# Bias part of a fused attention and MoE kernel: the fourth group of features of nine sets is made by GpSimd instead of VectorE

## The chip, the cores and the metric

The program runs on one core of one Trainium2 chip. The time is the device time of one execution in microseconds (us). The kernel is written engine by engine: each engine has its own instruction stream, and semaphores order them.

The names in the profile are PE for TensorE (PEld for its weight loads), DVE for VectorE, ACT for ScalarE, POOL for GpSimd and SP for the engine that only issues DMAs here.

## The reference

Three stages follow each other: attention with a learned bias by position, a dense layer pair, and a mixture of eight experts with one expert chosen per token. Only the first stage is touched:

```python
B, H, S, D = q.shape                       # 4, 8, 576, 64; hidden = 32
scores = scale * np.matmul(q, k.transpose(0, 1, 3, 2))
rel = (pos[:, None] - pos[None, :]).astype(np.float32)
psi_rel = np.log1p(np.abs(rel))
psi_i = np.log1p(np.maximum(pos[:, None].astype(np.float32), 1.0))
x = (psi_rel / psi_i)[..., None]
h = np.maximum(x @ w1 + b1, 0.0)           # 576 x 576 x 32
bias = h @ w2                              # 576 x 576 x 8
scores = scores + bias.transpose(2, 0, 1)[None, :, :, :]
```

The hidden layer h has 32 features for each pair of a query and a key, and is the same for all four batches. The softmax, the product with v, the dense stage and the experts follow.

## The kernel before

**What the bias part computes.** The 576 queries are cut in 36 sets of 16. A set has four groups of four queries. For one group, the 128 partitions hold 4 queries times 32 features, and the 576 columns are the keys. Since 1/psi_i is positive, it is taken out of the ReLU: a feature is max(w1 * psi_rel, -b1 * psi_i) plus a part that does not depend on the key, or relu(w1 * psi_rel + b1 * psi_i). The first form is one DVE tensor_scalar (a max against one number per partition, L630), the second one ACT activation (L543). Both read a window of 576 columns of the tile dist_sb (128x1148, f32) and write one of the four slots of a feature buffer feat, which has three buffers (NF = 3), 128x4x576 f32 each.

**Who makes which group.** DVE makes groups 0, 1 and 2 of each set (ACT_GROUP = 3). Group 3 is made by ACT in the sets where by_scalar(s) holds, s % 4 != 3, which are 27 sets, and by DVE in the other nine (s = 3, 7, ..., 35). So DVE makes 27*3 + 9*4 = 117 features.

**What follows a set.** TensorE multiplies the four slots by the 128x32 matrix w2_blk, 8 products of 288 columns (L401; the profile has each as two records, so a set is 16). It waits for feat_v (DVE's groups), for feat_a where ACT made one, and for acc_read, since the results alternate between two pairs of PSUM banks. ACT then scales the result into a row buffer (bias_rows, L553, for the last two sets L556), and SP stores it to DRAM (L332). The bias comes back from DRAM in tiles (L339) when the first scores of the attention need it.

**What sets the order.** Everything around the change is written out by hand, one loop over s per engine. DVE makes the features of set s after acc_ready says that TensorE has used the buffer of set s-3. ACT makes its group of set s+2 and then the rows of set s. Between sets, ACT and DVE also split the first k and q into high and low parts (L564; L639 and L642, five places). TensorE computes the first scores, scores(0, 0) at L420, between the last two sets. DVE then adds the bias to them (L657). GpSimd has no work in this part: its first own instruction is an indirect DMA of the routing, at 514.65 us of the span.

Of the kernel before, what the change touches and what calls it, by code (L numbers as in the profile page):

```python
# [23 lines left out]
ALU = mybir.AluOpType  # L24
# [16 lines left out]
SETS = S // SET  # L41
# [30 lines left out]
class Attention:  # L72
# [2 lines left out]
    tensor: object  # L75
    scalar: object
    vector: object
    over: object
    banks_read: object
    turned: object  # L80
# [73 lines left out]
def bias_and_attention(nc, stay, mem, w1, b1, w2, dist, psi, rpsi_rows, bias_dram, q, k, v, ident, x_dram):  # L154
# [7 lines left out]

    with ExitStack() as ctx:
        def sem(name):
            return stay.enter_context(nc.semaphore("at_" + name))

        def buf(name, shape, dt=F32):
            return ctx.enter_context(nc.sbuf_tensor("at_" + name, shape, dt))  # L170
# [6 lines left out]
        NF, NR = 3, 7  # L177
        ACT_GROUP = 3
        TILE_SETS = P // SET

        feat = [buf(f"feat{i}", [P, 4, S]) for i in range(NF)]
# [18 lines left out]
        lower, upper = buf("lower", [P, S // GQ]), buf("upper", [P, S // GQ])  # L200
# [14 lines left out]
        dist_scaled, b1_negated, bounds_set = sem("dist_scaled"), sem("b1_negated"), sem("bounds_set")  # L215
        shift_done, shift_zeroed, shift_read = sem("shift_done"), sem("shift_zeroed"), sem("shift_read")
        table_in = sem("table_in")
        feat_v, feat_a = sem("feat_v"), sem("feat_a")
        acc_ready, acc_read = sem("acc_ready"), sem("acc_read")
        rows_out = [sem(f"rows_out{i}") for i in range(NR)]  # L220

# [23 lines left out]
        def by_scalar(s):  # L245

            return s % 4 != 3

        def by_scalar_upto(s):

            return s + 1 - (s + 1) // 4

        def acc(s):

            if s < SETS - 2:
                return [score[s % 2][:, half, 0:HALF] for half in range(2)]
            return [bank[:, 0:HALF] for bank in ((pt_a, pt_b) if s == SETS - 2 else (o_acc, misc))]

        def window(s, c):
            return dist_sb[:, DIST0 - (4 * s + c) * GQ:DIST0 - (4 * s + c) * GQ + S]  # L260

        def column(t, s, c):
            return t[:, 4 * s + c:4 * s + c + 1]
# [125 lines left out]
        def tensor(pe, dense):  # L389
            def bias_set(s):  # L390
                pe.wait_ge(feat_v, s + 1)
                if by_scalar(s):
                    pe.wait_ge(feat_a, by_scalar_upto(s))
                if 2 <= s < SETS - 2:
                    pe.wait_ge(acc_read, s - 1)
                if s == SETS - 1:
                    pe.wait_ge(shift_read, 2)
                    pe.wait_ge(lo_done, NP)
                for half in range(2):
                    for c in range(4):  # L400
                        last = nc.tensor.matmul(acc(s)[half][c * 32:(c + 1) * 32, :], w2_blk[:, :],  # L401
                                                feat[s % NF][:, c, half * HALF:(half + 1) * HALF], start=True, stop=True)
                last.then_inc(acc_ready, 1)
# [78 lines left out]
            for s in range(SETS):  # L482
                bias_set(s)
                if s == SETS - 2:
                    scores(0, 0)
# [139 lines left out]
        def vector(dve, dense):  # L625
            def features(s):
                if s >= NF:
                    dve.wait_ge(acc_ready, s - NF + 1)
                for c in range(ACT_GROUP if by_scalar(s) else 4):
                    last = nc.vector.tensor_scalar(feat[s % NF][:, c, :], window(s, c), column(lower, s, c), None, ALU.max)  # L630
                last.then_inc(feat_v, 1)

# [85 lines left out]
            for s in range(SETS):  # L718
                features(s)
                if s - 4 in EARLY:  # L720
                    low(0, EARLY[s - 4])
# [39 lines left out]
            scaled(LASTP, 0, QT - 1, misc, 0)  # L761
            scaled(LASTP, QT - 1, 1, pt_a, 0)

        return Attention(sync, tensor, scalar, vector, over, banks_read, turned)

# [1269 lines left out]
def build(nc, io):  # L2037

    def scratch(name, shape, dt=F32):
        return nc.dram_tensor(name, shape, dt, kind="Internal").ap()  # L2040

    bias_dram = scratch("bias_dram", (S * NH, S))
    x_dram = scratch("x_dram", (DM, TOK))
    x2_dram = scratch("x2_dram", (TOK + 1, DM))
    slot_dram = scratch("slot_dram", (P * SLOT_COLS, 2), I32)
    with (nc.sbuf_tensor("ctl", [1, CTL], I32) as ctl, nc.sbuf_tensor("first_ctl", [1, 3 + NTT], I32) as first_ctl,
          nc.sbuf_tensor("slot_i", [P, NTT], I32) as slot_i, nc.sbuf_tensor("slot_rows", [P, NTT, 2], I32) as rows_sb):
        with ExitStack() as stay:
            def bank(name, shape):
                return stay.enter_context(nc.psum_tensor(name, shape, F32))  # L2050

            def buf(name, shape):
                return stay.enter_context(nc.sbuf_tensor(name, shape, F32))

            mem = Shared(buf("id_sb", [P, P]), stay.enter_context(nc.semaphore("id_in")),
                         [bank(f"score{c}", [P, 2, BANK]) for c in range(2)], bank("pt_a", [P, BANK]), bank("pt_b", [P, BANK]),
                         bank("misc", [P, BANK]), bank("o_acc", [P, BANK]), buf("minus_b", [P, 1]), buf("minus_small", [P, 1]),
                         buf("ones", [P, P]), buf("seen", [P, 2 * CH, NE]))
            first = bias_and_attention(nc, stay, mem, io["w1"], io["b1"], io["w2"], io["dist"], io["psi"], io["rpsi_rows"],
                                       bias_dram, io["q"], io["k"], io["v"], io["ident"], x_dram)  # L2060
            then = dense_and_routing(nc, stay, mem, first, ctl, first_ctl, slot_i, rows_sb, io["moe_w_in"], io["moe_w_out"],
                                     io["moe2_w_gate"], io["before"], io["token_ids"], io["down"], io["upto"],
                                     io["bases"], io["count"], io["empty"], io["zeros"], x_dram, x2_dram,
                                     slot_dram)
            last = experts(nc, stay, mem, then, ctl, first_ctl, io["moe2_w1"], io["moe2_w2"], x2_dram, slot_dram, io["out"])
            with nc.Block() as block:
                @block.sync
                def _(sp):
                    first.sync(sp, then)
                    then.sync(sp, last)  # L2070

                @block.tensor
                def _(pe):
                    first.tensor(pe, then)
                    then.tensor(pe, last)

                @block.scalar
                def _(act):
                    first.scalar(act, then)
                    then.scalar(act, last)  # L2080

                @block.vector
                def _(dve):
                    first.vector(dve, then)
                    then.vector(dve, last)

                @block.gpsimd
                def _(pool):
                    then.gpsimd(pool, last)


# [16 lines left out]
```

## Time and profile before

| | |
|---|---|
| median of 3 executions | 1054.19 us (1054.02 to 1054.94) |
| the profiled execution | 1053.72 us, of which the span of the profile is 1051.8 us |
| PE busy | 1012.9 us (96%) |
| DVE busy | 689.2 us (66%) |
| ACT busy | 631.2 us (60%) |
| POOL busy | 87.3 us (8%) |
| bias part | from the start to about 59.4 us of the span |

The span runs from the first to the last instruction of the profile; about 1.9 us of the execution lie outside it. The shares are means over stages that are limited by different engines. What the change is worth has to be read from the first 60 us, where TensorE is less busy than later and DVE more. Consecutive instructions of one engine overlap at their ends in the records (the next starts before the last one's results have landed), so the distance from start to start is shorter than the duration of one.

### The profile page before, as it was taken

How to read it: one execution, taken by the hardware profiler on the slowest of the kernel's cores; microseconds unless marked ns; L12 is line 12 of the kernel's file. 1: busy time of each engine (PE TensorE's matmuls, PEld its weight loads, DVE VectorE, ACT ScalarE, POOL GpSimd, SP SyncE). 2: the span in 40 equal slices, each digit the busy share in tenths (PEclk: the TensorE clock that was granted, in tenths of full speed). 3: DMA queues.
4: the chain of work that ended last, by engine and by line, in shares of the span. 5: the costliest groups of instructions: out<-in, count | busy, mean ns of one | idle time of the engine just before them, and what ended most of it. 6: DMA issues, size and time to landing. Idle time of an engine off the chain costs nothing. (4 is left out here: it accounts for less than half of the span.)

```text
span 1051.8 us, 19004 instructions
## 1 busy us (share of the span) xinstructions
PE 1012.9 (96%) x6540; PEld 787.9 (75%) x6540; DVE 689.2 (66%) x1570; ACT 631.2 (60%) x1340; POOL 87.3 (8%) x134
## 2 busy tenths in 40 slices
PE   6889999999999999999999999999998999999995
PEld 2256666666665789988988989888877888888884
DVE  7987878787888896766757657668754442632321
ACT  6987777777777685666566556567732432732421
POOL 0000000000000000000100100001023231331221
PEclk9999999999999999999999999999999999999998
DMA  7771252422512530010100100201115351631111
GB/s 227 265 250 56 71 168 71 160 81 65 148 46 94 183 111 1 31 31 31 31 1 31 31 1 31 81 31 58 40 51 205 122 195 40 215 102 40 36 40 36
DMA packets 62094, 92.15 MB, mean 88 GB/s; under 512 B 24486, under 2 KB 29990, under 8 KB 61990
## 3 DMA queue, kind: packets, MB, share of 16 engines
q1 hardware_dynamic: 56806, 79.32, 22.9%
q0 software_dynamic: 4192, 11.07, 3.3%
q8 instruction: 52, 0.85, 0.3%
q10 hardware_dynamic: 1008, 0.61, 0.2%
q14 instruction: 36, 0.29, 0.1%
HBM read 66.19 MB, written 25.73 MB: 87 GB/s over the span
## 5 line engine op out<-in xcount | busy, mean ns | idle before, releaser
L1009 PE MATMUL score<-dl_xt,dl_weights 128*128 128x384 f32 x1152 | 219.8, 339 | 0.0
L1009 PEld LDWEIGHTS score<-dl_xt,dl_weights 128*128 128x128 f32 x1152 | 202.1, 188 | 8.5 <-issue 3.0
L574 ACT ACTIVATE at_prob<-at_neg,at_negmax 128x576 f32<-128x576 f32 (+1 forms) x160 | 123.6, 773 | 54.2 <-DVE at_negmax L657 40.2
L1169 ACT ACTIVATE dl_val<-score 128x384 f32<-128x384 f32 x96 | 47.1, 490 | 131.3 <-PE score L1009 125.9
L1261 DVE SCALAR_TENSOR_TENSOR dl_sq<-dl_sq,dl_val 128x384 f32<-128x384 f32 x96 | 53.5, 557 | 99.3 <-ACT dl_sq L1171 97.7
L657 DVE CUSTOM_DVE_ANT_0 at_neg<-score,at_bias 128x576 f32<-128x576 f32 (+1 forms) x160 | 114.2, 750 | 2.2 <-PE score L420 1.7
L1814 PE MATMUL o_acc<-dl_weights,ex_ht_hi 128*128 128x512 f32 x336 | 109.1, 405 | 0.9 <-ACT ex_y_sb L1899 0.9
L1784 PE MATMUL score<-dl_weights,ex_xt_hi 128*128 128x512 f32 x336 | 105.6, 395 | 0.0
L435 PE MATMUL o_acc<-at_prob_t,at_v_nat 128*64 128x512 f32 (+1 forms) x320 | 85.7, 616 | 1.2 <-DVE at_o_sb L693 1.2
L428 PEld LDWEIGHTS pt_b<-id_sb,at_prob 128*128 128x128 f32 (+1 forms) x320 | 32.0, 140 | 63.5 <-ACT at_prob L574 48.1
L1479 POOL DMA_INDIRECT slot_dram<-slot_rows,slot_i x18 | 17.8, 987 | 727.5 <-DVE slot_i L1342 723.9
L1784 PEld LDWEIGHTS score<-dl_weights,ex_xt_hi 128*128 128x128 f32 x336 | 61.5, 188 | 12.2 <-issue 0.2
L1814 PEld LDWEIGHTS o_acc<-dl_weights,ex_ht_hi 128*128 128x128 f32 x336 | 60.0, 188 | 12.5 <-ACT ex_y_sb L1899 1.1
L1814 PE MATMUL o_acc<-dl_weights,ex_ht_lo 128*128 128x512 f32 x168 | 66.2, 394 | 0.0
L1784 PE MATMUL score<-dl_weights,ex_xt_lo 128*128 128x512 f32 x168 | 65.7, 391 | 0.0
L1054 PE MATMUL o_acc<-dl_weights,dl_g_hi 128*128 128x512 f32 x192 | 60.6, 396 | 1.9 <-DVE dl_g_lo L1257 1.6
L1171 ACT ACTIVATE dl_sq<-dl_val,minus_b 128x384 f32<-128x384 f32 x96 | 59.3, 618 | 3.1
L420 PE MATMUL score<-at_k_hi,at_q_hi 64*128 64x288 f32 x320 | 58.0, 340 | 2.6 <-DVE at_negmax L657 2.0
L1272 DVE COPY_PREDICATED dl_sq<-dl_over,dl_big 128x384 f32<-128x384 uint32 x96 | 57.8, 602 | 3.5 <-DVE dl_sq L1268 0.2
L1054 PE MATMUL score<-dl_weights,dl_g_hi 128*128 128x512 f32 x192 | 59.8, 392 | 0.0
L1054 PE MATMUL pt_b<-dl_weights,dl_g_hi 128*128 128x512 f32 x192 | 59.3, 390 | 0.0
L1179 ACT ACTIVATE dl_over<-dl_val,minus_small 128x384 f32<-128x384 f32 x96 | 58.2, 606 | 0.0
(222 smaller groups left out, 1985.8 us busy)
## 6 DMA issues: line engine op xcount, KB each, us to landing
dl_raw<-in_moe_w SPq DMA_DIRECT2D x12, 1024.0 KB, 7.6
ex_raw_b<-in_moe_w SPq DMA_DIRECT2D x8, 1024.0 KB
at_bias<-bias_dram SPq DMA_DIRECT2D x3, 2304.0 KB, 10.2
bias_dram<-at_prob SPq DMA_DIRECT2D x20, 288.0 KB, 2.1
at_k_all<-in_k SPq DMA_DIRECT2D x16, 288.0 KB, 3.5
at_q_all<-in_q SPq DMA_DIRECT2D x16, 288.0 KB, 4.2
at_v_nat<-in_v SPq DMA_DIRECT2D x16, 288.0 KB, 3.1
bias_dram<-at_rows_sb SPq DMA_DIRECT2D x16, 288.0 KB, 3.6
```

The lines of the kernel that those rows point to most:

```text
L420: last = nc.tensor.matmul(score[c][:, half, 0:HALF], a[g % 2][part, cols], b[g % 2][part, keys], start=i == 0, stop=i == 2)
L435: last = nc.tensor.matmul(o[c * D:(c + 1) * D, at:at + queries.stop - queries.start], v_nat[g % NV][keys, j, :], prob_t[g % 2][keys, j, qu ...
L574: nc.scalar.activation(prob[n % 2][0:m, c, :], neg[c][n % 2][0:m, :], ACT.Exp, bias=negmax[c][n % 2][0:m, 0:1], scale=-1.0, accum_out=tota ...
L657: nc.vector.tensor_tensor_reduce(out=neg[c][n % 2][0:m, :].rearrange("p (a c) -> p a c", a=2), in0=score[c][0:m, :, 0:HALF], in1=bias[hp % ...
L1009: last = nc.tensor.matmul(h_ps[m % NHB][:, 0:CN], w[f // KT][:, k, fc], x[c % 2][:, k, :], start=k == 0 and n == 0, stop=k == KT - 1 and n ...
L1054: last = nc.tensor.matmul(x2_ps[j][:, :], g[m % 2][:, tok], w[f // KT][:, f % KT, :], start=f == 0 and n == 0, stop=f == FT - 1 and n == 2)
L1171: nc.scalar.activation(sq[m % 2][:, :], val[m % 2][:, :], ACT.Square, bias=minus_b[:, 0:1], scale=SQ_A).then_inc(sq_done, 1)
L1179: nc.scalar.activation(over[m % 2][:, :], val[m % 2][:, :], ACT.Relu, bias=minus_small[:, 0:1]).then_inc(over_done, 1)
L1261: nc.vector.scalar_tensor_tensor(out=sq[m % 2][:, :], in0=sq[m % 2][:, :], scalar=SQ_C, in1=val[m % 2][:, :], op0=ALU.add, op1=ALU.mult).t ...
L1272: nc.vector.copy_predicated(s[:, :], over[m % 2][:, :].bitcast(mybir.dt.uint32), big[m % 2][:, :]).then_inc(dve_step, 1)
L1784: last = nc.tensor.matmul(h_ps[half][:, :], x[:, k, :], w1_of(r, half, w)[:, k, :], start=k == 0 and n == 0, stop=k == KT - 1 and n == 2)
L1814: last = nc.tensor.matmul(y_ps[:, :], x[:, half * KT + k, :], weights[:, r % 2, half, w, k, :], start=half == 0 and k == 0 and n == 0, sto ...
```

## The change

GpSimd gets an instruction stream for the bias part. In the nine sets of which ACT makes no group, it makes group 3, by the same tensor_scalar with the same operands that DVE had. DVE makes three groups of every set. TensorE waits for a new semaphore, feat_g, in these nine sets. GpSimd waits for the same two semaphores at the start as DVE, and for acc_ready before it writes to a buffer that was used before, which all nine were.

```diff
-        feat_v, feat_a = sem("feat_v"), sem("feat_a")
+        feat_v, feat_a, feat_g = sem("feat_v"), sem("feat_a"), sem("feat_g")
...
                 pe.wait_ge(feat_v, s + 1)
                 if by_scalar(s):
                     pe.wait_ge(feat_a, by_scalar_upto(s))
+                else:
+                    pe.wait_ge(feat_g, s + 1 - by_scalar_upto(s))
...
-                for c in range(ACT_GROUP if by_scalar(s) else 4):
+                for c in range(ACT_GROUP):
                     last = nc.vector.tensor_scalar(feat[s % NF][:, c, :], window(s, c), column(lower, s, c), None, ALU.max)
                 last.then_inc(feat_v, 1)
...
+        def gpsimd(pool):
+
+            pool.wait_ge(dist_scaled, 1)
+            pool.wait_ge(bounds_set, 2)
+            for s in range(SETS):
+                if not by_scalar(s):
+                    if s >= NF:
+                        pool.wait_ge(acc_ready, s - NF + 1)
+                    nc.gpsimd.tensor_scalar(feat[s % NF][:, ACT_GROUP, :], window(s, ACT_GROUP), column(lower, s, ACT_GROUP), None,
+                                            ALU.max).then_inc(feat_g, 1)
...
                 def _(pool):
+                    first.gpsimd(pool)
                     then.gpsimd(pool, last)
```

On DVE, in sets 0 to 5 of the bias part, the program before has these rows (at_feat0 to at_feat2 are the three feature buffers; x2 stands for two in a row):

```order
L630 TENSOR_SCALAR at_feat0<-at_dist_sb,at_lower 128x576 [waits at_bounds_set,at_dist_scaled]
L630 TENSOR_SCALAR at_feat0<-at_dist_sb,at_lower 128x576 x2
L630 TENSOR_SCALAR at_feat1<-at_dist_sb,at_lower 128x576 x3
L630 TENSOR_SCALAR at_feat2<-at_dist_sb,at_lower 128x576 x3
L630 TENSOR_SCALAR at_feat0<-at_dist_sb,at_lower 128x576 [waits at_acc_ready]
L630 TENSOR_SCALAR at_feat0<-at_dist_sb,at_lower 128x576 x3
L630 TENSOR_SCALAR at_feat1<-at_dist_sb,at_lower 128x576 [waits at_acc_ready]
L630 TENSOR_SCALAR at_feat1<-at_dist_sb,at_lower 128x576 x2
```

The same place on DVE in the changed program:

```order
L634 TENSOR_SCALAR at_feat0<-at_dist_sb,at_lower 128x576 [waits at_bounds_set,at_dist_scaled]
L634 TENSOR_SCALAR at_feat0<-at_dist_sb,at_lower 128x576 x2
L634 TENSOR_SCALAR at_feat1<-at_dist_sb,at_lower 128x576 x3
L634 TENSOR_SCALAR at_feat2<-at_dist_sb,at_lower 128x576 x3
L634 TENSOR_SCALAR at_feat0<-at_dist_sb,at_lower 128x576 [waits at_acc_ready]
L634 TENSOR_SCALAR at_feat0<-at_dist_sb,at_lower 128x576 x2
L634 TENSOR_SCALAR at_feat1<-at_dist_sb,at_lower 128x576 [waits at_acc_ready]
L634 TENSOR_SCALAR at_feat1<-at_dist_sb,at_lower 128x576 x2
```

Set 3, the second use of at_feat0, has three instructions now where it had four, and the same holds for each fourth set after it. On GpSimd the changed program has, between the constants at its start and the first DMA of the routing, which stood next to each other before:

```order
L2113 MEMSET const-uint8-127 128x1
L2102 UNCONDITIONAL_BRANCH [waits barrier_Pool_Activation_PE_DVE_SP_gather]
L776 ISA
L776 TENSOR_SCALAR at_feat0<-at_dist_sb,at_lower 128x576 [waits at_acc_ready,at_bounds_set,at_dist_scaled]
L776 TENSOR_SCALAR at_feat1<-at_dist_sb,at_lower 128x576 [waits at_acc_ready]
L776 TENSOR_SCALAR at_feat2<-at_dist_sb,at_lower 128x576 [waits at_acc_ready]
```

Nine instructions moved there, for sets 3, 7, 11 and so on, with nothing else between them. On TensorE only the wait of set 3 and its like changes; before, sets 3 and 4 begin with

```order
L401 MATMUL score1<-at_feat0,at_w2_blk 32x288 [waits at_acc_read,at_feat_v]
L401 MATMUL score1<-at_feat0,at_w2_blk 32x288 x7
L401 MATMUL score0<-at_feat1,at_w2_blk 32x288 [waits at_acc_read,at_feat_a,at_feat_v]
L401 MATMUL score0<-at_feat1,at_w2_blk 32x288 x7
L401 MATMUL score1<-at_feat2,at_w2_blk 32x288 [waits at_acc_read,at_feat_a,at_feat_v]
```

and in the changed program with

```order
L405 MATMUL score1<-at_feat0,at_w2_blk 32x288 [waits at_acc_read,at_feat_g,at_feat_v]
L405 MATMUL score1<-at_feat0,at_w2_blk 32x288 x7
L405 MATMUL score0<-at_feat1,at_w2_blk 32x288 [waits at_acc_read,at_feat_a,at_feat_v]
L405 MATMUL score0<-at_feat1,at_w2_blk 32x288 x7
L405 MATMUL score1<-at_feat2,at_w2_blk 32x288 [waits at_acc_read,at_feat_a,at_feat_v]
```

The products of set 3 wait for GpSimd too; no instruction of TensorE moves.

## Rows read from the trace of the kernel before

**Rows 1.** Stretches of the span: busy us (instructions) by engine, clock, DMA

```profile
14.00:24.00 10.00, 8.90 (x128) 3.81 (x120) 10.00 (x24) 10.00 (x15) 0.00 (x0) 1.00 0.60 227
24.00:57.00 33.00, 26.44 (x365) 9.56 (x366) 33.00 (x81) 30.50 (x48) 0.00 (x0) 1.00 0.76 258
```

**Rows 2.** Waits, 24 to 57 us: total, times, longest us

```profile
PEld score L401 <- DVE at_feat L630: 18.8, 23, 1.4
PE score L401 <- DVE at_feat L630: 5.1, 10, 0.8
```

**Rows 3.** Timeline of DVE, bias part: start, us, instruction, count, idle before

```profile
6.85 3.95 DVE L630 TENSOR_SCALAR at_feat<-at_dist_sb,at_lower 128x576 f32<-128x576 f32 x9
11.29 22.41 DVE L630 TENSOR_SCALAR at_feat<-at_dist_sb,at_lower 128x576 f32<-128x576 f32 x52 [0.49 <-PE score L401]
33.62 0.42 DVE L639 TENSOR_TENSOR at_k_lo<-at_k_all,at_k_hi 128x256 fp32r<-128x256 f32 x1
...
52.03 7.40 DVE L630 TENSOR_SCALAR at_feat<-at_dist_sb,at_lower 128x576 f32<-128x576 f32 x17
59.97 0.76 DVE L657 CUSTOM_DVE_ANT_0 at_neg<-score,at_bias 128x576 f32<-128x576 f32 x1 [0.54 <-PE score L420]
```

**Rows 4.** Timeline of ACT, from the rows of set 1 to set 5

```profile
12.72 0.83 ACT L553 ACTIVATE at_prob<-score,at_shift,at_rows_scale 128x576 f32<-128x576 f32 x1 [0.60 <-PE score L401]
...
17.71 0.83 ACT L553 ACTIVATE at_rows_sb<-score,at_shift,at_rows_scale 128x576 f32<-128x576 f32 x1
```

**Rows 5.** Timeline, TensorE and ACT, a set's products and the last full rows

```profile
21.45 1.18 PE L401 MATMUL score<-at_feat,at_w_blk 128*32 128x288 f32 x16 [0.21 <-ACT at_rows_sb L553]
...
57.73 0.83 ACT L553 ACTIVATE at_rows_sb<-score,at_shift,at_rows_scale 128x576 f32<-128x576 f32 x1 [0.36 <-PE score L401]
```

**Rows 6.** Groups by shape, 0 to 75 us: busy us, mean ns | idle before

```profile
L630 DVE TENSOR_SCALAR at_feat<-at_dist_sb,at_lower 128x576 f32<-128x576 f32 x117 | 50.9, 518 | 0.5 <-PE score L401 0.5
L543 ACT ACTIVATE at_feat<-at_dist_sb,at_upper 128x576 f32<-128x576 f32 x27 | 20.6, 765 | 1.2 <-DVE at_dist_sb L715 1.2
L639 DVE TENSOR_TENSOR at_k_lo<-at_k_all,at_k_hi 128x256 fp32r<-128x256 f32 x4 | 1.7, 422 | 1.5 <-ACT at_k_hi L564 1.5
L564 ACT ACTIVATE at_k_hi<-at_k_all 128x256 fp32r<-128x256 f32 x4 | 1.7, 413 | 0.0
L715 DVE TENSOR_SCALAR at_dist_sb<-at_dist_sb,at_w1c 128x1148 f32<-128x1148 f32 x1 | 0.8, 814 | 0.0
L639 DVE TENSOR_TENSOR at_k_lo<-at_k_all,at_k_hi 128x64 fp32r<-128x64 f32 x2 | 0.5, 226 | 0.8 <-ACT at_q_hi L564 0.8
```

**Rows 7.** Groups by shape on POOL, whole span

```profile
L1685 POOL COPY dl_tile_rows<-ex_slots_sb 128x1 f32 x19 | 3.3, 173 | 0.0
L1685 POOL COPY dl_tile_rows<-dl_x_nat 128x1 f32 x2 | 0.7, 364 | 0.0
```

**Rows 8.** Timeline of POOL, 839 to 850 us

```profile
841.26 0.85 POOL L1684 COPY dl_tile_rows<-ex_slots_sb 128x1 int32 x1 [2.62 <-DMA out<-ex_y_sb,dl_tile_rows]
842.06 0.17 POOL L1685 COPY dl_tile_rows<-ex_slots_sb 128x1 f32 x1
843.53 1.38 POOL L1676 COPY dl_tile_rows<-ex_slots_sb 128x1 int32 x1 [1.30 <-issue]
845.72 2.81 POOL L1679 DMA_INDIRECT ex_x_sb<-x_dram,dl_tile_rows  x1 [0.81 <-POOL dl_tile_rows L1676]
```

**Rows 9.** Timeline of DVE, 839 to 850 us

```profile
839.78 2.29 DVE L1939 TENSOR_TENSOR dl_weights<-ex_raw_b,dl_weights 128x2048 fp32r<-128x2048 f32 x1 [1.84 <-ACT dl_weights L1860]
841.99 0.68 DVE L1965 TENSOR_SCALAR ex_h_sb<-score 128x512 f32<-128x512 f32 x1
842.59 2.28 DVE L1939 TENSOR_TENSOR dl_weights<-ex_raw_b,dl_weights 128x2048 fp32r<-128x2048 f32 x1
...
845.39 4.49 DVE L1939 TENSOR_TENSOR dl_weights<-dl_raw,dl_weights 128x2048 fp32r<-128x2048 f32 x2
```

**Rows 10.** Timeline of POOL, 901 to 925 us

```profile
908.15 2.81 POOL L1679 DMA_INDIRECT ex_x_sb<-x_dram,dl_tile_rows  x1 [0.81 <-POOL dl_tile_rows L1676]
912.46 1.02 POOL L1691 DMA_INDIRECT out<-ex_y_sb,dl_tile_rows  x1 [1.51 <-ACT ex_y_sb L1899]
```

More of the change, by code:

```diff
@@ L77 @@
     vector: object
+    gpsimd: object
     over: object
@@ L762, in vector @@
             scaled(LASTP, QT - 1, 1, pt_a, 0)
-        return Attention(sync, tensor, scalar, vector, over, banks_read, turned)
+        def gpsimd(pool):
[7 more added lines that the diff above has]
+                                            ALU.max).then_inc(feat_g, 1)
+        return Attention(sync, tensor, scalar, vector, gpsimd, over, banks_read, turned)
 FF = 2048
```

## The prediction, made before the changed kernel was run

> **What bounds the kernel now.** I read the busy shares of stretches first, then the waits, then the timeline of the busiest engine. In the bias part DVE is busy in all of the 43 us from 14 to 57 us of the span [rows 1]. ACT is busy in all of the first ten of them and in 30.50 of the other 33. PE is busy in 35.34. The waits say who sets the pace: from 24 us on PE and its weight loads wait for DVE's features, and for nothing else that adds up [rows 2]. The timeline of DVE shows it without a gap [rows 3]: 52 features stand in one run from 11.29 to 33.62 us, which is 22.33/52 = 0.429 us from start to start, and the next idle time is 0.54 us before 59.97, when the first bias is added to the scores. The granted clock is 1.00 in both stretches, so the clock plays no part. After the bias part comes the attention, which begins when scores, bias and DVE are there. All of that moves with the end of the features, and I take it to shift whole. So a microsecond on DVE before 59.4 us is a microsecond of the kernel, for as long as DVE stays the bound.
>
> **Part 1: DVE loses nine features.** 9 x 0.429 = 3.87 us less on the engine that sets the pace. Nothing hides it. What is late next is ACT: from the rows of set 1 at 12.72 to those of set 5 at 17.71 it has no gap and takes 4.99 us for four sets [rows 4]. From set 1 to set 33 that is 8 x 4.99 = 39.9 us. With the seven splits of k and q among them, at 0.413 us for the 128x256 form [rows 6] and less for the smaller ones, some 2.2 us in all, the rows of set 33 could start at 12.72 + 39.9 + 2.2 = 54.8. They start at 57.73 [rows 5]. So ACT lets at most 2.9 us of the 3.87 through at that point. Some of the rest comes back in the last sets. I put the gain of this part at 2.9 to 3.9 us if nothing is paid for it.
>
> **Part 2: GpSimd makes nine features, and what one takes.** No row has an elementwise instruction of this size on POOL. From below: it needs at least what DVE needs from start to start, 0.43 us. From the nearest rows: a COPY of one column takes 0.173 us [rows 7], which I take as the fixed part. The part per column I take from the engines that do one element at a time. DVE's L639 goes from 226 to 422 ns for 192 more columns, 1.02 ns each. ACT goes from 413 to 765 ns for 320 more, 1.10 ns each [rows 6]. 576 columns at that are 0.59 to 0.63 us, so one feature is about 0.79 us. From above: twice the time per column, 0.17 + 1.2 = 1.4 us. I take 0.79, which is nearest to the rows of plain one-input work.
>
> **Part 3: whether that lies beside DVE's work.** This decides the sign. DVE's feature instruction is fast in a particular way: 576 columns take 518 ns and 1148 columns take 814 ns [rows 6], 0.52 ns per column, half of the 1.02 ns that L639 shows. It moves two elements at a time. The trace also has a place where POOL meets DVE. At 841.26 a POOL COPY of one column takes 0.85 us instead of 0.17, and ends at 842.11. The DVE subtraction that it fell into, which reads two tiles of the on-chip memory, ends at 839.78 + 2.29 = 842.07 [rows 8, 9]. The next COPY begins at 843.53 and ends at 844.91; DVE's next such subtraction ends at 844.87. Eight COPYs of the trace are stretched to 0.79 to 1.90 us, each until about 0.04 us after the end of such an instruction. The COPY at 842.06, beside a DVE instruction that reads from PSUM, takes its 0.17. So POOL waits for a whole DVE instruction that uses the second way into the memory, and for no other. That feature instructions at twice the rate use it too is what their rate suggests. That DVE in its turn waits while POOL works is not seen, since POOL's copies are too short to show it.
>
> The Trainium skill, "SBUF — State Buffer", section "Who interferes with whom", states both: a DVE instruction in a two-port mode and a GpSimd instruction exclude each other, whoever starts first holds the ports for its whole length, and the other is blocked fully. By that rule, each POOL feature would stand in DVE's way for all of its length. The trace agrees in one direction (the COPY that waits until 842.11) and is silent on the other.
>
> I take exclusion in both directions as the likeliest. Then the two engines' features stand in one row, and the change swaps 0.43 us of DVE for the whole POOL feature. To its 0.79 us I add the overlap that DVE loses at the hand-over: an instruction lasts 0.518 but the next starts after 0.429, so 0.09. That is 0.88 - 0.43 = 0.45 us more for each of nine, 4.0 us in all. The bounds of part 2 give 9 x (0.43 + 0.09 - 0.43) = 0.8 us and 9 x (1.4 + 0.09 - 0.43) = 9.5 us.
>
> The Trainium skill, "GPSIMD Engine Reference", section "3.1 Elementwise — side-by-side cycle accounting", gives 769 ns for 512 elements at 1.8 cycles each. As an estimate that is 865 ns for 576, and the sum would be 4.7 us instead of 4.0. No run here shows it.
>
> **Part 4: the waits that are added.** POOL starts its feature of set s when TensorE is through with set s-3, and nothing is queued behind it there: its next own work is at 514 us. TensorE needs it at set s, about three sets later. A set is 13 x 0.429 / 4 = 1.39 us on DVE and 1.18 us of products [rows 5], so POOL has some 3 x 1.39 - 1.18 = 3.0 us. It needs at most one DVE instruction of waiting and its own 0.8, so feat_g is there in time. Cost: nothing. If POOL took over 2.5 us, TensorE would wait for it with the sets behind it, and ACT's rows behind those. SP has the same DMAs as before.
>
> **The sum.** The profiled execution took 1053.72 us, 0.47 below the median of 1054.19. With 4.0 it would be 1057.7; against the median 1058.2. I state 1058.2.
>
> **The rivals.** *A, no exclusion where it matters.* POOL and DVE run beside each other. For it: the trace has no DVE instruction that waits for POOL, and only instructions with two inputs are seen to hold POOL up. Against it: the doubled rate of L630. Then part 1 stands alone: 2.9 to 3.9, I take 3.2, so 1051.0 us. It decides from the point where POOL holds DVE for under 0.43 us per feature.
>
> *B, exclusion, but for about as long as it saves.* POOL needs the ports only while columns stream, and its start and end lie outside. At 0.45 to 0.6 us held, the net is under 2 us: 1054.2 to 1056.
>
> *C, POOL gets no turn while DVE's features follow each other without a gap.* DVE starts each instruction before the last one has ended, so it may keep the ports until it stops for a full ring, three sets on. Then POOL's 0.8 us, a set of products of 1.18 us and two semaphores of about 0.2 us stand in a row, 2.3 us for 0.43, in eight or nine sets: some 15 us, 1069 us. Against it: at 845.72 POOL's indirect DMA lasts 2.81 us, beside two subtractions that follow each other directly. It ends at 848.53, which is 0.86 us after the end of the first (845.39 + 2.28 = 847.67) and before the end of the second at 849.88 [rows 8, 9]. The one at 908.15 lasts the same, and one that DVE doesn't disturb 1.02 us [rows 10]. So POOL gets its turn between two DVE instructions.
>
> **How the numbers follow.** What this kernel's measurement can tell from no change is about 0.2%, 2.1 us. Exclusion with 2.1 us or more: 0.54. B, or exclusion near its lower bound: 0.17. A: 0.23. C, or a first POOL instruction that is slow once (its first float COPYs took 0.364 us in the mean instead of 0.173 [rows 7], so little): 0.06. So faster 0.23, within 0.2% 0.17, slower 0.60. The forecast itself runs from 1055 to 1063.7, its bounds. A has more than two in ten, so the range must take it in: from 1050.5 to 1063.5. It leaves out C and the tails.
>
> **What would show it.** In the profile after, the bias part ends near 63.4 us instead of 59.4 and the add of L657 starts there. DVE's run of 52 features is 48 now, with stalls of 0.8 to 0.9 us beside each POOL instruction, as longer durations or as larger distances from start to start. POOL shows nine instructions of 0.8 us or, with waiting for ports, up to 1.3. If A holds, DVE's distance stays 0.429 all along, ACT has no gap, and DVE begins to wait for acc_ready. The prediction falls if POOL's instruction is much under 0.5 us, if DVE's instructions beside it are not stretched, or if the attention behind does not shift whole.

## The result: 0.73% slower, 1062.4 us

| | before | after |
|---|---|---|
| median | 1054.38 us (4 runs, 1054.02 to 1054.94) | 1062.39 us (4 runs, 1062.13 to 1063.02) |
| profiled execution, span | 1053.72, 1051.8 us | 1062.56, 1060.7 us |
| first bias add of the attention starts at | 59.97 us | 68.35 us |

The ratio is 1.0073, with a 95% interval of 1.0061 to 1.0085. The medians are 8.0 us apart, where 4.0 were forecast: inside the range, 1.1 us below its upper end, and on the forecast side. Of the 8.9 us by which the span grew, 8.38 are there at the first add of a bias (L657 before, L661 after). The bias part is where the time went.

GpSimd's part of the timeline of the changed kernel holds the surprise. Six of its nine features are shown (start, us, instruction, idle before it and what ended that):

```profile
17.38 2.61 POOL L776 TENSOR_SCALAR at_feat<-at_dist_sb,at_lower 128x576 f32<-128x576 f32 x1 [3.47 <-PE score L405]
22.52 2.57 POOL L776 TENSOR_SCALAR at_feat<-at_dist_sb,at_lower 128x576 f32<-128x576 f32 x1 [2.53 <-PE score L405]
28.47 6.66 POOL L776 TENSOR_SCALAR at_feat<-at_dist_sb,at_lower 128x576 f32<-128x576 f32 x1 [3.38 <-PE score L405]
39.10 2.69 POOL L776 TENSOR_SCALAR at_feat<-at_dist_sb,at_lower 128x576 f32<-128x576 f32 x1 [3.97 <-PE score L405]
44.16 2.63 POOL L776 TENSOR_SCALAR at_feat<-at_dist_sb,at_lower 128x576 f32<-128x576 f32 x1 [2.37 <-PE score L405]
50.17 5.52 POOL L776 TENSOR_SCALAR at_feat<-at_dist_sb,at_lower 128x576 f32<-128x576 f32 x1 [3.38 <-PE score L405]
```

Seven of the nine features take 2.2 to 2.7 us, and two take 6.66 and 5.52. DVE answers in two ways. The first is that single instructions are stretched. In narrow stretches of DVE's timeline, two of them near the GpSimd feature of 17.38 are:

```profile
18.12 0.92 DVE L634 TENSOR_SCALAR at_feat<-at_dist_sb,at_lower 128x576 f32<-128x576 f32 x1
...
19.39 0.91 DVE L634 TENSOR_SCALAR at_feat<-at_dist_sb,at_lower 128x576 f32<-128x576 f32 x1
```

Between them stands one of normal length. All the others in that stretch last 0.51. So DVE is held up twice per GpSimd feature, by 0.40 us each time, 0.80 in all, and makes a feature of its own in between. The durations of the feature instructions (shortest, median, longest in ns) and their group by shape show the same over the whole part:

```profile
L634 DVE TENSOR_SCALAR at_feat<-at_dist_sb,at_lower x108: 500/508/1002, 6.9 to 67.3; 128x576 f32<-128x576 f32 x108
L634 DVE TENSOR_SCALAR at_feat<-at_dist_sb,at_lower 128x576 f32<-128x576 f32 x108 | 53.7, 569 | 5.8 <-PE score L405 5.7
```

The mean is 569 where the median is 508: 108 x 0.061 = 6.6 us of being held up. That is 0.81 for each of eight GpSimd features; the ninth, of 28.47, held up none. The end of the second line is the second answer: 5.7 us of idle time in which DVE waits for TensorE, where it had 0.5 before [rows 6]. DVE's timeline, 28 to 38 us, and TensorE's, 35 to 37 us, show where most of it is:

```profile
28.32 5.23 DVE L634 TENSOR_SCALAR at_feat<-at_dist_sb,at_lower 128x576 f32<-128x576 f32 x12
37.44 0.95 DVE L634 TENSOR_SCALAR at_feat<-at_dist_sb,at_lower 128x576 f32<-128x576 f32 x2 [3.89 <-PE score L405]
```

```profile
35.23 2.15 PE L405 MATMUL score<-at_feat,at_w_blk 128*32 128x288 f32 x16 [4.32 <-POOL at_feat L776]
```

Beside the GpSimd feature that started at 28.47, none of DVE's twelve instructions is stretched (5.23 us for 12, 0.429 from start to start as before). GpSimd gets nowhere while they follow each other. At 33.55 DVE has filled the three buffers and stops. Then GpSimd runs, and ends at 35.13, 1.58 us later. TensorE has waited for it for 4.32 us. Its products of that set then take 2.15 us and not 1.18 [rows 5], since TensorE runs at a granted clock of 0.50, that is 1.2 GHz, as the stretches show (the last three numbers are clock, DMA share and GB/s):

```profile
35.20:37.40 2.20, 2.17 (x20) 1.13 (x24) 0.00 (x0) 0.00 (x0) 0.00 (x0) 0.50 0.00 0
46.60:49.00 2.40, 1.78 (x28) 0.55 (x24) 2.40 (x7) 2.29 (x5) 0.19 (x1) 1.00 0.73 269
55.60:58.00 2.40, 2.21 (x20) 1.13 (x24) 1.26 (x4) 0.00 (x1) 0.09 (x1) 0.50 0.78 282
```

So the 3.89 us in which DVE is idle are 1.58 of GpSimd, 2.15 of products and 0.16 between them.

The same happens at 50.17, less badly. TensorE stands for 2.70 us, its products take 2.15 again, and DVE is idle for 1.14 us. Without the lower clock each of the two idle times would be 2.15 - 1.18 = 0.97 us shorter; as an estimate from these rows, 1.9 of their 5.0 us are the clock.

The account of the bias part is then: 9 x 0.43 = 3.87 us taken off DVE, 6.6 us of being held up, 5.7 - 0.5 = 5.2 us of idle time more, and 0.06 us of later start (DVE's first feature starts at 6.91, before at 6.85). That is 8.0 of the 8.38 us. A third stretch at half clock, at 806.6 to 809.8 us, stands in the part behind, where the span gained the other 0.5 us; such a stretch occurs in some of the profiles below and not in others, and I put no more weight on it.

### The profile page after: what moved, and what is told of

The parts are those of the page before. It is cut to its first block and busy times, and to the rows that moved or that the text cites. A ratio compares the mean times of both kernels' runs of the same rounds, so it can differ in the third digit from the quotient of the medians.

```text
span 1060.7 us, 19008 instructions
## 1 busy us (share of the span) xinstructions
PE 1017.7 (96%) x6540; PEld 791.4 (75%) x6540; DVE 692.0 (65%) x1561; ACT 631.5 (60%) x1340; POOL 118.0 (11%) x143
## 5 line engine op out<-in xcount | busy, mean ns | idle before, releaser
L661 DVE CUSTOM_DVE_ANT_0 at_neg<-score,at_bias 128x576 f32<-128x576 f32 (+1 forms) x160 | 114.1, 749 | 2.5 <-PE score L424 2.0
```

The costliest lines, as they stand in the source:

```text
L661: nc.vector.tensor_tensor_reduce(out=neg[c][n % 2][0:m, :].rearrange("p (a c) -> p a c", a=2), in0=score[c][0:m, :, 0:HALF], in1=bias[hp % ...
```

## Experiments

The theory after these rows: (1) the two engines exclude each other on the ports to the on-chip memory, for 0.80 us of DVE per GpSimd feature; (2) GpSimd can be shut out altogether while DVE's features follow each other, and then TensorE, and with it DVE, stand still, at half clock afterwards. The rival: GpSimd is just too slow, and TensorE's wait for it costs the time.

**The held ports alone.** All 117 features stay on DVE. GpSimd makes its nine in addition, into a tile that nobody reads.

```diff
+                if g == 0 and t == 1:
+                    dve.wait_ge(pool_done, 9)
...
+            for s in range(SETS):
+                if not by_scalar(s):
+                    pool.wait_ge(acc_ready, s - NF + 1)
+                    nc.gpsimd.tensor_scalar(unread[:, 0:576], window(s, ACT_GROUP)[:, 0:576], column(lower, s, ACT_GROUP), None, ALU.max).then_inc(pool_done, 1)
+                    pool.wait_ge(pool_done, 0 + s // 4 + 1)
```

> The kernel before (DVE makes all its 117 features), and GpSimd in addition makes the same nine instructions at the same points, into a tile that nobody reads; nothing in the bias part waits for it. Theory (the ports are the cost: each GpSimd feature holds DVE up twice for 0.40 us, 0.81 in all, as the trace of after shows at 18.1 and 19.4 us): 7 to 9 times 0.81, so 5.7 to 7.3 us more than before, 1060 to 1061.7, and DVE instructions of 0.91 us in pairs. Rival (GpSimd is only slow, 2.2 to 6.7 us per feature, and what costs is TensorE's wait for feat_g): nobody waits here, so 1054.4, unchanged.

Measured: 1062.41 us against 1054.74, ratio 1.0065 (1.0049 to 1.0082). The expected 1060 to 1061.7 was a little low; the rival's 1054.4 is out. Nobody waits for GpSimd in the bias part here, and yet it costs 7.7 us. (DVE's one wait for it stands behind the bias part, and the idle time before DVE's add there is 1.21 us, as without it.) DVE has no more idle time than before; its instructions are longer:

```profile
L633 DVE TENSOR_SCALAR at_feat<-at_dist_sb,at_lower 128x576 f32<-128x576 f32 x117 | 57.3, 561 | 0.5 <-PE score L404 0.5
```

The first bias add starts at 66.95, 6.98 us later than before, of which 0.46 are a later start (11.75 for 11.29 us). The other 6.5 fall on eight GpSimd features, 0.81 each: the ninth ran when DVE's features were over. GpSimd's and DVE's timelines show two more things:

```profile
17.42 20.17 POOL L775 TENSOR_SCALAR at_unread<-at_dist_sb,at_lower 128x576 f32<-128x576 f32 x1 [3.29 <-PE score L404]
63.56 4.45 POOL L775 TENSOR_SCALAR at_unread<-at_dist_sb,at_lower 128x576 f32<-128x576 f32 x1 [4.31 <-PE score L404]
```

```profile
34.97 0.41 DVE L642 TENSOR_TENSOR at_k_lo<-at_k_all,at_k_hi 128x256 fp32r<-128x256 f32 x1
35.31 1.77 DVE L633 TENSOR_SCALAR at_feat<-at_dist_sb,at_lower 128x576 f32<-128x576 f32 x3
...
66.95 0.76 DVE L660 CUSTOM_DVE_ANT_0 at_neg<-score,at_bias 128x576 f32<-128x576 f32 x1 [0.53 <-PE score L423]
```

The GpSimd feature that started at 17.42 took 20.17 us, since DVE never ran dry here. It got in behind the first DVE instruction that was not a feature, L642 at 34.97: of the three features after it one is stretched (1.77 us for three, where 1.37 is normal), and GpSimd ends at 37.59. In the changed kernel the feature of 50.17 got in the same way, behind L646 at 53.07. And the last one ended at 68.01 beside L660, which reads one operand from PSUM and one from SBUF, and lasts 0.76 as it does before [rows 3]: that form is not held up.

**The work taken off, alone.** The nine features are made by nobody; in nine sets TensorE multiplies what an earlier set left in the fourth slot, so the bias of those sets is not computed right.

```diff
-                for c in range(ACT_GROUP if by_scalar(s) else 4):
+                for c in range(ACT_GROUP):
```

> The nine features that moved are made by nobody: DVE makes three groups of each set, and in nine sets TensorE multiplies what stands in the fourth slot from an earlier set, so the bias of those sets is another one. It prices the first part of the sum alone, the work taken off DVE. Theory (DVE sets the pace and ACT lets 2.9 us through at set 33): 2.9 to 3.9 us less, 1050.5 to 1051.5. Rival (ACT or TensorE is so close behind DVE that little is won): under 1.5 us less.

Measured: 1052.09 us against 1054.74, ratio 0.9972 (0.9962 to 0.9981), 2.65 us less. The first bias add starts at 57.37, 2.60 us earlier. That is a little under the expected 2.9 to 3.9. ACT had not quite the room that the count gave it: it is busy in 30.78 of the 31 us behind 24 us.

```profile
24.00:55.00 31.00, 26.78 (x380) 11.55 (x372) 31.00 (x76) 30.78 (x49) 0.00 (x0) 1.00 0.84 287
```

**Letting GpSimd in.** The changed kernel with one DVE memset of one column after the features of each set.

```diff
                 last.then_inc(feat_v, 1)
+                nc.vector.memset(gap[:, s:s + 1], 1.0)
```

> The changed kernel, with one DVE memset of a single column after the three features of each set. Theory (GpSimd got no turn in two of nine cases because DVE's two-port instructions follow each other without a gap, and a small instruction that doesn't hold the shared ports gives it one): all nine GpSimd features take 2.7 us or less, DVE is never idle for TensorE, the clock stays at full speed. Time: 9 x (0.81 - 0.43) = 3.4 for the ports and 36 memsets of about 0.06 to 0.1, 2.2 to 3.6, so 1059.9 to 1061.4. Rival (what shuts GpSimd out is something else, such as its own start): one to three features of 5 to 7 us remain, and the memsets come on top of 1062.4, so 1064 to 1066.

Measured: 1058.80 us against 1054.74, ratio 1.0038 (1.0026 to 1.0051): by the two ratios some 3.7 us faster than the changed kernel, with more instructions. The forecast of 1059.9 at the least was too high by a microsecond, since the memsets overlap with the features: three features and a memset take 1.30 us from start to start, three features alone 3 x 0.429 = 1.29. GpSimd's and DVE's features:

```profile
L778 POOL TENSOR_SCALAR at_feat<-at_dist_sb,at_lower x9: 2150/2245/2592, 11.6 to 59.9; 128x576 f32<-128x576 f32 x9
```

```profile
L635 DVE TENSOR_SCALAR at_feat<-at_dist_sb,at_lower x108: 500/509/1000, 7.0 to 62.8; 128x576 f32<-128x576 f32 x108
L635 DVE TENSOR_SCALAR at_feat<-at_dist_sb,at_lower 128x576 f32<-128x576 f32 x108 | 54.5, 576 | 0.5 <-PE score L406 0.5
```

None of the nine is over 2.6 us, DVE is idle 0.5 us as before the change, and no stretch of the bias part is at half clock. What is left is the held time: 108 x (0.576 - 0.509) = 7.2 us, 0.80 per feature. 7.2 - 3.87 = 3.4. The first bias add starts 3.88 us later than before (63.85); 0.12 of the other 0.5 us are there when DVE's long run of features starts (11.41 for 11.29), and some 0.3 are the 36 memsets. So the 8.0 us split into about 4 of ports and about 4 of late features.

**How few of them it takes.** The memset only after the sets with s % 4 == 1, nine in all.

```diff
                 last.then_inc(feat_v, 1)
+                if s % 4 == 1:
+                    nc.vector.memset(gap[:, s:s + 1], 1.0)
```

> The changed kernel with nine small memsets instead of 36: one after the features of each set with s % 4 == 1, two sets before the one that GpSimd works for, so about 0.4 to 1 us before or after GpSimd's start. If a single small instruction near GpSimd's start is what lets it in: all nine at 2.7 us or less, no idle time of DVE, 9 x (0.80 - 0.43) = 3.3 us more than before, 1057.5 to 1058.8. If it took the small instruction in every set (because it breaks up the run of features as a whole): one to three long GpSimd features, 1059.5 to 1063.

Measured: 1058.59 us against 1054.84, ratio 1.0032 (1.0019 to 1.0044). All nine GpSimd features take 2.13 to 2.61 us. One small instruction near GpSimd's start was enough. (Seven of nine got in without one in the changed kernel, so nine of nine here would be weak evidence alone.)

**Whether it must be an instruction of another kind.** The memset is replaced by a tensor_scalar of two columns, SBUF to SBUF, the form of the features.

```diff
-                nc.vector.memset(gap[:, s:s + 1], 1.0)
+                nc.vector.tensor_scalar(gap[:, 2 * s:2 * s + 2], upper[:, 2 * s:2 * s + 2], 1.0, None, ALU.mult)
```

> As the kernel with the small memset after each set, but the small instruction is a DVE tensor_scalar of two columns from SBUF to SBUF, the same form as the features. Theory (GpSimd is shut out as long as DVE instructions that hold the shared ports follow each other): the small one holds them too, so one to three GpSimd features of 4 to 7 us come back, with DVE idle and a clock at half speed, 1062 to 1067. Rival (any small instruction, by its delay of some 0.03 us or by being short, lets GpSimd in): all nine at 2.7 us or less, 1059 to 1061.

Measured: 1060.06 us against 1054.69, ratio 1.0051 (1.0035 to 1.0066).

```profile
L778 POOL TENSOR_SCALAR at_feat<-at_dist_sb,at_lower x9: 2190/2432/2616, 11.7 to 61.6; 128x576 f32<-128x576 f32 x9
```

No feature is late. The theory expected late ones, and this part of it falls: the small instruction need not be of another form to let GpSimd in. Being short, or the change that it makes to DVE's rhythm, is enough. Being short isn't needed either: L642, which let GpSimd in above, lasts 0.41 us. These 36 small instructions add 0.07 us each from start to start where a memset adds 0.01. That is 2.2 us in all, as the two profiled executions differ; the medians differ by 1.3.

**More slack.** GpSimd gets two buffers of its own and may run five sets further ahead.

```diff
+        def group_at(s, c):
+            return feat[s % NF][:, c, :] if c < ACT_GROUP or by_scalar(s) else ahead[s // 4 % 2]
...
-                                                feat[s % NF][:, c, half * HALF:(half + 1) * HALF], start=True, stop=True)
+                                                group_at(s, c)[:, half * HALF:(half + 1) * HALF], start=True, stop=True)
...
-                    if s >= NF:
-                        pool.wait_ge(acc_ready, s - NF + 1)
-                    nc.gpsimd.tensor_scalar(feat[s % NF][:, ACT_GROUP, :], window(s, ACT_GROUP), column(lower, s, ACT_GROUP), None,
+                    if s >= 8:
+                        pool.wait_ge(acc_ready, s - 8 + 1)
+                    nc.gpsimd.tensor_scalar(ahead[s // 4 % 2], window(s, ACT_GROUP), column(lower, s, ACT_GROUP), None,
```

> The changed kernel, but GpSimd writes its features to two buffers of its own and may run five more sets ahead (it waits for set s-8 instead of s-3). Ports are shared as before, but a feature that gets no turn has some 7 us more before TensorE needs it. Theory (about 3.4 us are ports, the other 5 are the two features that came late, with the clock that fell behind them): long GpSimd instructions may remain but nobody waits for them, 1057.5 to 1058.5. Rival (the whole loss is ports): 1061 or more, as before the move.

Measured: 1060.97 us against 1054.74, ratio 1.0059 (1.0042 to 1.0075). I expected 1058, and missed. The time is about the rival's, but its mechanism is not: DVE has an idle time of 3.89 us. The timelines of GpSimd and DVE say why:

```profile
15.19 13.11 POOL L780 TENSOR_SCALAR at_ahead<-at_dist_sb,at_lower 128x576 f32<-128x576 f32 x1 [3.81 <-PE score L409]
28.28 1.71 POOL L780 TENSOR_SCALAR at_ahead<-at_dist_sb,at_lower 128x576 f32<-128x576 f32 x1
```

```profile
16.75 9.96 DVE L638 TENSOR_SCALAR at_feat<-at_dist_sb,at_lower 128x576 f32<-128x576 f32 x23
30.60 1.87 DVE L638 TENSOR_SCALAR at_feat<-at_dist_sb,at_lower 128x576 f32<-128x576 f32 x3 [3.89 <-PE score L409]
```

The slack was eaten. DVE ran on undisturbed until its buffers were full, and the feature took 13.11 us. A second late one, of 5.25 us at 54.34, cost DVE no idle time with the slack, so the slack took away the smaller of the two waits.

Being shut out has no length of its own: it lasts until DVE stops or does something else. This holds for all 13 GpSimd instructions that were shut out in the traces of the changed kernel, of this one, and of the three with unread output (one above, two below). Five ran once DVE had stopped. The other eight got in behind the first DVE instruction that was not a feature, all of them two-input splits of k or q of 0.28 to 0.42 us. Slack only moves the stop. With the memsets as well, the slack should then add nothing.

> Own buffers for GpSimd's features (five sets of slack more) together with the 36 small memsets. If the memsets take away all late features and only the held ports are left, the slack adds nothing: the time of the kernel with the memsets alone, 1058 to 1059.5. If GpSimd's latency of 2.2 to 2.6 us still cost something without the slack: 1 us or more below that.

Measured: 1058.42 us against 1054.84, ratio 1.0032 (1.0020 to 1.0043), beside 1.0038 and 1.0032 for the two kernels with memsets and without the slack. It adds nothing, so GpSimd's own 2.2 to 2.6 us cost nobody anything.

**What a hold is.** Two more kernels, both with all features on DVE and GpSimd's output unread: GpSimd instructions of 288 columns, and memsets of 576 columns, with two undisturbed tensor_scalars at the start.

```diff
-                    nc.gpsimd.tensor_scalar(unread[:, 0:576], window(s, ACT_GROUP)[:, 0:576], column(lower, s, ACT_GROUP), None, ALU.max).then_inc(pool_done, 1)
+                    nc.gpsimd.tensor_scalar(unread[:, 0:288], window(s, ACT_GROUP)[:, 0:288], column(lower, s, ACT_GROUP), None, ALU.max).then_inc(pool_done, 1)
```

The other one, against the same kernel:

```diff
+            for i in range(2):
+                nc.gpsimd.tensor_scalar(unread[:, :], unread[:, :], 1.0, None, ALU.max).then_inc(pool_done, 1)
...
-                    nc.gpsimd.tensor_scalar(unread[:, 0:576], window(s, ACT_GROUP)[:, 0:576], column(lower, s, ACT_GROUP), None, ALU.max).then_inc(pool_done, 1)
+                    nc.gpsimd.memset(unread[:, 0:576], 1.0).then_inc(pool_done, 1)
```

> As the first experiment (all 117 features on DVE, nine GpSimd instructions that nobody reads), with 288 columns instead of 576 in each GpSimd instruction. What holds DVE up: if the ports are held while columns stream, each of the two holds falls from 0.40 to about 0.2 us (DVE instructions of 0.7 us); if a hold is a fixed price of an instruction, it stays 0.40 and DVE instructions stay 0.91.

> The nine GpSimd instructions in the bias part only write (memset of 128x576, nobody reads it), and two GpSimd tensor_scalars of 128x576 run at the start, while DVE waits for its first load. Theory (one hold for reading, one for writing, or both in pieces): the memset holds DVE up too, by 0.4 to 0.8 us each. Rival (only a GpSimd instruction that reads SBUF meets DVE): no stretched DVE instruction, time as before. The two at the start give the undisturbed length of a GpSimd feature: 1.3 to 1.8 us if the 2.2 to 2.6 us are its own work and DVE's turns between, 2.2 if they are all its own.

The first took 1056.58 us and the second 1057.10, each in one execution; the reading rests on the durations in their profiles. DVE instructions beside the halves, and beside the memsets:

```profile
34.74 0.67 DVE L633 TENSOR_SCALAR at_feat<-at_dist_sb,at_lower 128x576 f32<-128x576 f32 x1
```

```profile
17.39 0.92 DVE L633 TENSOR_SCALAR at_feat<-at_dist_sb,at_lower 128x576 f32<-128x576 f32 x1
```

With 288 columns a hold is 0.67 - 0.51 = 0.16 us instead of 0.40: it grows by 0.24/288 us, 0.83 ns per column, between these two sizes, so it fits ports that are taken while columns stream, and not a fixed price. It comes twice per tensor_scalar there too. A memset, which only writes, makes one hold of 0.41. So each of the two holds of a feature may be one pass over its columns; this is an inference, and so is that one of the two is its reading and the other its writing. The memset is shut out as well: the first of the three at 22.25 takes 12.88 us. GpSimd's timeline of that kernel:

```profile
0.80 0.58 POOL L770 MEMSET at_unread<- 128x576 f32 x1 [0.29 <-POOLq L2117]
1.48 3.39 POOL L773 TENSOR_SCALAR at_unread<-at_unread 128x576 f32<-128x576 f32 x2
...
22.25 14.53 POOL L780 MEMSET at_unread<- 128x576 f32 x3 [4.26 <-PE score L404]
```

The two undisturbed tensor_scalars at the start take 3.39 us, 1.7 each. So does the feature of 28.28 in the kernel with own buffers, 1.71 us while DVE stood. So 1.7 is GpSimd's own work, and the 2.2 to 2.6 us of the bias part hold waits for DVE's turns.

**Another engine for the same work.** No GpSimd; ScalarE makes the fourth group in 30 sets instead of 27.

```diff
-            return s % 4 != 3
+            return s % 6 != 5
...
-            return s + 1 - (s + 1) // 4
+            return s + 1 - (s + 1) // 6
```

> The kernel before with no GpSimd work, ScalarE making the fourth group in 30 sets (s % 6 != 5) instead of 27 and DVE in 6. DVE loses 3 features, 1.3 us; ACT gains 3, at 0.67 us each 2.0, out of the 2.9 us by which it was ahead at set 33. If DVE's count sets the time: 0.9 to 1.3 us less, 1053.4 to 1053.9. If ACT becomes the bound: no change or up to 1 us more.

Measured: 1054.62 us against 1054.69, ratio 0.9997 (0.9988 to 1.0006): no change. The stretches of its profile (busy us of PE, PEld, DVE, ACT, POOL) have both engines full:

```profile
14.00:24.00 10.00, 8.88 (x132) 3.92 (x128) 9.92 (x24) 9.86 (x15) 0.00 (x0) 1.00 0.56 209
24.00:57.00 33.00, 27.62 (x384) 10.01 (x376) 33.00 (x81) 32.37 (x51) 0.00 (x0) 1.00 0.78 267
```

ACT, which had 2.5 us of idle time there before [rows 1], has 0.8. So the kernel before was close to balanced between the two. No kernel here that makes all the features is faster than it.

## Why the prediction was right, step by step, and what was mis-sized

The sign was right, and so was the main mechanism, the exclusion. That the time lies inside the range is in part luck. About half of the 8 us is a wait that the sum had at nothing, and two errors in the other half cancel: a GpSimd feature takes twice the forecast time, but holds DVE up for only half of it. The whole 1.7 us held would have given 9 x (1.7 + 0.09 - 0.43) = 12.2 us, outside the range.

- **What bounds the kernel.** Right. DVE's features set the pace, and the attention shifted whole: 8.38 of 8.9 us were there at the first bias add.
- **Part 1, the work taken off.** 3.2 us was taken for it alone, 2.65 measured. ACT was nearer than counted.
- **Part 2, what a GpSimd feature takes.** Mis-sized. It takes 1.7 us undisturbed, not 0.79, and lies above the upper bound of 1.4 and the 865 ns of the other estimate. With its waits for ports it takes 2.2 at the least, where up to 1.3 was given as a sign. Taking DVE's and ACT's time per column for GpSimd's and its one-column copy for the fixed part was no basis.
- **Part 3, exclusion.** Right in both directions, and by the form that was named: the DVE features are stretched, L660 is not. The price was nearly right for a wrong reason. 0.88 us of DVE per feature was forecast, 0.80 measured, but not as one whole instruction: a GpSimd feature holds DVE up for 2 x 0.40 us, and takes 1.7. The sum of parts 1 and 3 was 4.0; with the late features taken away it measured 3.8 to 4.1 (1058.6 and 1058.8), of which the memsets are some 0.3 us.
- **The page on who holds the ports.** The Trainium skill, "SBUF — State Buffer", section "Who interferes with whom", has the exclusion right, and DVE instructions of 0.91 us instead of 0.51 confirm it. It says that the ports are held for the whole instruction. The trace differs: DVE made a whole feature between two holds, and a 1.7 us instruction cost it 0.80.
- **Part 4, the waits.** Wrong. That the feature is there in time, at no cost, holds for seven features and for all nine where the memsets stand; two came late, and they cost the other half of the 8 us. The point from which TensorE would wait was given as 2.5 us, and they took 5.5 and 6.7. (TensorE waited for GpSimd twice more, for 0.6 us at the most, and DVE did not stop for it.) The step that failed is "It needs at most one DVE instruction of waiting": beside the feature of 28.47 twelve went by.
- **Rival C, GpSimd gets no turn.** Put at 0.06 with others and dismissed on indirect DMAs that got in between two long subtractions. Those subtractions are instructions with two inputs, and behind such ones (L642, L646) GpSimd got in here as well; it is between features that it did not. The rival was true in two of nine cases. It happened beside the main case and not instead of it, which the chances had no room for. A case was priced at 2.3 us; the two left DVE idle for 3.89 and 1.14 us. The first is over the price since GpSimd took 1.58 us for 0.8 and the products 2.15 for 1.18.
- **The clock.** "Plays no part" was wrong for the kernel after: when TensorE stood still for 4.32 us, the granted clock was 0.50 afterwards, and the set that everyone waited for took 2.15 us instead of 1.18.

## What to carry to other kernels

In this kernel GpSimd was no spare engine beside a VectorE that runs one-input f32 instructions from SBUF to SBUF at 0.52 ns per column, half of the 1.02 that the two-input L639 takes: 576 columns moved there saved 0.43 us of VectorE and cost it 0.80. Where VectorE read from PSUM, it was not held up in the one case seen (L660), so such work may fit there; that was not tried. If something of GpSimd's must run beside a dense row of such instructions and someone waits for it, put a short VectorE instruction near it (nine memsets of one column won back about half of the 8 us here). More buffers alone did not do it: 1.0059 for 1.0073, with intervals that overlap. An instruction of another kind that VectorE has to make anyway, such as the split of k here, served as well.

## What the runs showed of the hardware

- A GpSimd tensor_scalar of 128x576 f32 takes 1.7 us undisturbed and a memset of that size 0.58. Beside VectorE's features the first held VectorE up twice for 0.40 us, the second once for 0.41; at 288 columns a hold was 0.16.
- A GpSimd instruction was shut out by VectorE features that start every 0.429 us for as long as they followed each other: 6.66, 13.11 and 20.17 us were seen for one instruction. It ended in all 13 cases when VectorE stopped (five) or made one instruction that was not a feature (eight). In other cases with the same rhythm GpSimd got in after 0.7 us. What decides that is open. In the four kernels with short VectorE instructions among the features (memsets of one column in three, tensor_scalars of two columns in one) all 36 GpSimd features took 2.7 us or less. Shortness isn't what it takes, since a two-input instruction of 0.41 us did it as well; whether it is a shift of phase was not tried.
- After TensorE had stood still for 4.32 us the granted clock was 0.50, that is 1.2 GHz, in the stretch from 35.20 to 37.40 us, and 1.00 again in the one from 46.60 on. The same came after a stand of 2.70 us (55.60 to 58.00). With the unread output it was 0.50 from 38.30 to 41.50, after a stand of 1.64 us, and DVE had no more idle time for it.
